# Fused attention and two feed-forward layers on one core: the order of VectorE's products with h and the lower parts of weights, and one W_out part on GpSimd

## The reference

```python
def _moe_ref(x, w_in, w_out):                 # layer 0
    h = x @ w_in
    g = h * np.clip(h + 3.0, 0.0, 6.0) / 6.0
    return (g @ w_out).astype(np.float32)

def _moe2_ref(x, w_in, w_out):                # layer 1
    h = x @ w_in
    sp = np.where(h > 20.0, h, np.log1p(np.exp(np.minimum(h, 20.0))))
    return ((h * np.tanh(sp)) @ w_out).astype(np.float32)

def reference(q, k, v, moe_w_in, moe_w_out, moe2_w_in, moe2_w_out):
    attn_out = _attn_ref(q, k, v)             # 4 x 8 heads, 576 x 64, block-causal softmax
    x = attn_out.transpose(0, 2, 1, 3).reshape(2304, 512)
    x = _moe_ref(x, moe_w_in, moe_w_out)      # 512 -> 2048 -> 512
    return _moe2_ref(x, moe2_w_in, moe2_w_out)
```

## Time and profile before

| | |
|---|---|
| median of 3 runs | 978.65 us (973.37 to 980.71) |
| the profiled execution | 975.95 us |
| its span | 974.0 us |
| TensorE busy | 952.0 us, 98% of the span |
| VectorE, ScalarE, GpSimd busy | 746.6, 643.6, 431.3 us |

### The profile page before, as it was taken

The page is one execution under the profiler, slowest core; times in us unless marked ns, Lnnn a source line. Parts: engine busy times, 40 slices in busy tenths (PEclk is TensorE's granted clock), DMA queues, the critical chain, the costliest instruction groups (busy, mean ns, idle before and its releaser), DMA issues.

```text
span 974.0 us, 17754 instructions
## 1 busy us (share of the span) xinstructions
PE 952.0 (98%) x6028; PEld 848.0 (87%) x6028; DVE 746.6 (77%) x1417; ACT 643.6 (66%) x1431; POOL 431.3 (44%) x410
## 2 busy tenths in 40 slices
PE   8999999999999999999899999999999999999998
PEld 7898888999887888888788988998998988988896
DVE  7898898774868686789788787777887777777654
ACT  7999999754544445454445557777777777776663
POOL 7899779665837596776867670000000000000000
PEclk9999999999999999999999999999999999999999
DMA  7988898657698978788786546555655654565255
GB/s 217 270 240 243 258 273 234 173 153 238 220 291 291 290 256 252 234 294 252 269 275 212 209 170 217 176 202 195 215 197 184 231 210 155 182 248 187 90 193 194
DMA packets 84601, 216.42 MB, mean 222 GB/s; under 512 B 10144, under 2 KB 16928, under 8 KB 84512
## 3 DMA queue, kind: packets, MB, share of 16 engines
q1 hardware_dynamic: 84368, 215.01, 67.6%
q10 hardware_dynamic: 144, 0.29, 0.1%
HBM read 162.07 MB, written 39.92 MB: 207 GB/s over the span
## 4 chain that ended last, share of the span: by engine, by line
PE 67%; DVE 7%; DMA 6%; SPq 4%; POOL 3%; issue 2%; ACT 1%; ACTq 0%; DVEq 0%; POOLq 0%
PE psum L1021 32%; PE psum L904 10%; PE psum L906 10%; PE psum L905 10%; DMA ext_d<-ext_made 3%; PE psum L849 2%; PE psum L828 2%; DVE ebuf L1624 1%; PE psum L808 1%; POOL osplit L1885 1%; SPq L646 1%; DVE glo L1630 1%; PE psum L809 1%; SPq L648 1%; DVE ext_made L1530 1%
## 5 line engine op out<-in xcount | busy, mean ns | idle before, releaser
L1021 PE MATMUL psum<-ghi,osplit 128*128 128x512 f32 (+1 forms) x640 | 216.7, 372 | 2.1 <-POOL osplit L1885 2.1
L904 PE MATMUL psum<-xhi,whi 128*128 128x256 f32 (+1 forms) x640 | 188.0, 294 | 5.1 <-ACT snap L1242 2.5
L906 PE MATMUL psum<-xhi,wlo 128*128 128x256 f32 (+1 forms) x640 | 187.2, 293 | 0.0
L905 PE MATMUL psum<-xlo,whi 128*128 128x256 f32 (+1 forms) x640 | 187.0, 292 | 0.0
L1021 PE MATMUL psum<-osplit,ghi 128*128 128x512 f32 x576 | 180.7, 395 | 1.3 <-DVE glo L1630 1.3
L1630 DVE SCALAR_TENSOR_TENSOR glo<-ebuf,ghi 128x512 fp32r<-128x512 f32 x144 | 126.5, 878 | 22.9 <-ACT ghi L1290 14.8
L904 PEld LDWEIGHTS psum<-xhi,whi 128*128 128x128 f32 x640 | 121.1, 189 | 19.0 <-ACT snap L1242 4.4
L1290 ACT ACTIVATE ghi<-ebuf 128x512 fp32r<-128x512 f32 x144 | 90.4, 628 | 66.9 <-DVE ebuf L1624 46.2
L1021 PEld LDWEIGHTS psum<-ghi,osplit 128*128 128x128 f32 x640 | 118.5, 190 | 18.4 <-issue 2.7
L1885 POOL TENSOR_TENSOR osplit<-oraw,osplit 128x512 fp32r<-128x512 f32 x80 | 117.2, 1468 | 38.1 <-ACT osplit L1209 34.0
L905 PEld LDWEIGHTS psum<-xlo,whi 128*128 128x128 f32 x640 | 121.2, 189 | 10.5
(11 more groups left out here) (120 smaller groups left out, 2147.4 us busy)
## 6 DMA issues: line engine op xcount, KB each, us to landing
ext<-ext_d SPq DMA_DIRECT2D x56, 768.0 KB, 4.4
osplit<-o_d SPq DMA_DIRECT2D x80, 512.0 KB, 5.3
oraw<-in_w_out SPq DMA_DIRECT2D x80, 256.0 KB, 5.8
wraw<-in_w_in SPq DMA_DIRECT2D x26, 512.0 KB, 6.0
ext_d<-ext_made SPq DMA_DIRECT2D x32, 384.0 KB, 6.2
attn_t<-ostage SPq DMA_DIRECT2D x32, 288.0 KB, 3.7
qkin<-in_qk SPq DMA_DIRECT2D x30, 288.0 KB, 3.7
kparts<-kparts SPq DMA_DIRECT2D x30, 288.0 KB, 4.2
```

The source lines that it names most:

```text
L904: pe.matmul(dst, hi, xh, start=(start and cc == 0), stop=False, skip_group_check=True)
L905: pe.matmul(dst, hi, xl, start=False, stop=False, skip_group_check=True)
L906: last = pe.matmul(dst, lo, xh, start=False, stop=(stop and cc == 1), skip_group_check=True)
L1021: last = pe.matmul(bank(Y_BANK + c, n), stat, mov, start=(first and m == 0), stop=(final and m == 2), skip_group_check=True)
```

## The change

VectorE: in `relu_period(s)` the two calls `extra_jobs(s - 1)` and `ahead_os(s - 1)` move behind both products with h and behind the low part of g of the first of the two tiles. GpSimd: in step 0 `mix_x(1, 1)`, the last sum of x for the wide block, moves behind the second `split_o`, that of tile 4. No instruction is added or taken away, and no wait is changed.

```diff
                 if first_of_block(s):
                     copy_y(BLOCK_OF[s] - 1, 3)
-                extra_jobs(s - 1)
-                ahead_os(s - 1)
                 relu6_times_h(s + 1, 0)
                 relu6_times_h(s + 1, 1)
                 split_g_lo(s + 1, 0)
+                extra_jobs(s - 1)
+                ahead_os(s - 1)
                 mixing_jobs(s)
...
                 if s == 0:
                     add_x(1, 3)
                     scale_x(1, 3)
-                    mix_x(1, 1)
                 next_x(s, 0)
                 for i in todo[1:2]:
                     split_o(i)
+                if s == 0:
+                    mix_x(1, 1)
                 next_x(s, 1)
```

## The result

The changed kernel takes 981.84 us in the median of 12 runs (978.29 to 983.53), the kernel before 975.73 us in 12 runs beside it (973.28 to 980.71). The ratio is 1.0066 with a 95% interval of 1.0050 to 1.0082: slower by 6.4 us, surely slower than before, and within the 1% that I took as no change. 982 was forecast. One further execution of the kernel before, in a later batch, took 1536 us at a granted clock of 0.557 and is in no ratio. The profiled spans are 974.0 us before and 979.5 us after, +5.5.

The account below looks back on a forecast made before the run. TensorE, busy in 98% of the span, bounds the kernel; its relevant waits are 10.3 us. Terms -3.6 + 2.8 + 2.7 - 1.8 + 3.7 + 0 = +3.8 us on the 978.65 median give 982; range 970 to 990.

Parts of the forecast that it names:

- Part 1: GpSimd in step 0: tile 4's low part before the mixing ends TensorE's 2.1 us wait and the low clock: -3.6 us.
- Part 2: VectorE's products earlier: waits for snap5, product and snap_3 end; -1.8 us before step 14, -4.9 in steps 20 to 26.
- Part 3: W_out loads in step 3: tile 16's load starts 6.9 us later, delaying copy_y and TensorE's bank: +2.8 us.
- Part 4: x loads in step 6: lower parts end 2.9 us later, so x reaches TensorE late; cover 0.2: +2.7 us.
- Part 5: x loads in step 14: released 4.15 us later, with nothing to cover it: +3.7 us, bounds 2.2 and 4.2.
- Part 6: x loads in step 22 come 3.3 us later, TensorE 1.9 later; with 2.0 won earlier kept, net about 0.
- Rival B: New long waits let TensorE's clock drop, 1.6 us each: up to 993 us; chance 0.23 beyond 1%, 0.2 inside.
- Rival A: TensorE's waits go and nothing takes their place: -10.4 to -11.4 us, 967 to 968; chance beyond 1% 0.12.
- Rival C: Only GpSimd's half shows; parts 3 to 6 come to what part 2 gives: -3.6, so 975 us; chance 0.2.
- the signs named in the forecast: snap5, snap_3 and step 0 waits gone; three x waits, some 10 us; x loads 3 and 4 us later; SyncE waits grow.
- theory 2: From the experiments, not the prediction: the order itself costs; the sums or the W_out tiles come late whenever x lands.

Follow-up runs that it names:

- run 1: Kernel before with only GpSimd's half: in step 0 the last x sum for the wide block moves behind tile 4's split; ratio 1.0016, 975.27 us.
- run 2: Kernel before with only VectorE's half: the lower parts of extra operands and W_out behind the products with h; ratio 1.0081, 982.24 us.
- run 9: Kernel before with ten one-element loads ahead of the x loads in steps 6, 14 and 22, no buffer added; ratio 1.0016, 976.48 us.
- run 10: Kernel before with ten one-element loads ahead of the W_in and W_out loads in steps 6, 14 and 22; ratio 1.0051, 980.34 us.
- Run 6: Changed kernel with VectorE's two lower parts between the first and second half's products with h; ratio 0.9969 to the kernel before, 974.03 us.
- run 11: Kernel before with VectorE's lower parts between the two halves' products with h, GpSimd's step 0 as before; ratio 0.9982, 973.71 us.
- run 12: Kernel before with one unused 16-element buffer ahead of the others, no instruction changed; ratio 1.0063, 981.32 us.
- run 8: Kernel before with an added 16-element buffer and five one-element loads ahead of the x loads in steps 6, 14 and 22; ratio 1.0051.

## Why the prediction was right, and where it was not

The time and its class came out: 982 forecast, 981.84 measured, and a shift of +6.4 us by the ratio where the sum said +3.8. Part of that is luck. First, the frame: the forecast was put on a median of 978.65 us from three executions, and the 12 beside the changed kernel have 975.73. The base was 2.9 us too high and the shift 2.6 us too small; on the later base the same sum gives 979.5. Second, several terms were off and made up for each other. What was right is the direction and the path: lower parts late on VectorE, SyncE's queue held up, x late, TensorE's first products of a block waiting for it.

- **Part 1, GpSimd in step 0: -3.6 forecast, -1.7 measured.** Mis-sized. Tile 4's low part no longer stood behind the mixing, but ScalarE's high part of tile 4 (L1209) ran only at 209.27, and TensorE waited 0.95 us for tile 4 and 0.37 for tile 5. "Nearly all goes, since 2.33 is more than 2.1" asked only for the old obstacle; I should have looked for the one behind it. And by runs 1 and 2 the gain is neither GpSimd's own nor one that lasts.
- **Part 2, the products earlier.** Of the -4.9 of steps 20 to 26, 2.0 were forecast to be won by step 22 and to stay: 1.4 was won from step 19 to 22, 1.95 to step 24. Of the -1.8 before step 14 the small one came (0.56 in step 12); the wait of 1.5 us for the first product (L1624) only shrank to 1.0.
- **Part 3, W_out loads in step 3: +2.8 forecast, +0.46 measured.** Mis-sized. Tile 16's load started at 241.17, not 242.8, and ScalarE could use it at 244.43, 3.3 us later. I had taken the page's median of 5.8 for a moment when the DMA engines were nearly idle (a share of 0.02 from 239.0 to 241.2); in the changed kernel that median itself is 4.8. The bound of 0.8 was not low enough.
- **Part 4, x loads in step 6: +2.7 forecast.** The low part of x came 2.1 us later where 2.9 was forecast, and TensorE lost 3.3 us in step 9 (from -1.22 to +2.04), since it arrived earlier. Another 2.04 us went in step 10 to the second wait and the slow clock, of which 0.56 came back in step 12. The size was about right, the cause half so: x was late because the W_in and W_out loads ahead of it were (runs 9 and 10), not because of its own issue. In the changed kernel both move together, which is why the sum came out.
- **Part 5, x loads in step 14: +3.7 forecast, +2.9 measured**, and of those a wait of 2.62 us and the slow clock behind it. x was 3.0 us later against the step where 4.15 was forecast.
- **Part 6, step 22: +1.9 forecast, +1.0 measured** (from step 24 to 28). x was 4.2 us later against the step where 3.3 was forecast, and the sum given for it, 4.4 less 1.3, is itself 3.1. The waits of 2.00 and 1.55 us stand where one of 4.8 was expected.
- **Rival B** was not a rival but a part of what happened. I gave the forecast no drops, and one or two of them a chance of 0.2. There were three stretches, one of them of double length, behind three of the four new long waits. Less the one of before that went, they made 3.7 of the 5.5 us. The Trainium skill's rule cited there ("TensorE: Matmul & The Clock Gate", section "What's actually happening"), that idleness brings the slow clock back, is borne out: the new stretches stand at waits of 3.02, 2.62 and 2.00 us, and none at that of 1.55. The wait of 2.32 us in the earlier trace rows had none, so the length of a single wait doesn't settle it.
- **Rival A** would have needed the lower parts to be free of followers. Run 6 is what is left of A: with the lower parts as early as before and one product in front, it is 0.3% faster.
- **Rival C**, that only GpSimd's half shows, is refuted by run 1, in which that half alone brought nothing.

What the signs named in the forecast showed: x loads 3.6 us later in step 6 and 3.0 in step 14 against the step (3 and 4 were named), SyncE's waits for VectorE grown, three waits for x (7.2 us where some 10 were named). The waits for snap_3 did not go; there is one of 2.00 us at 484.28, and it is the new order's own. VectorE's lower part had waited 1.55 us for its buffer and began at 477.23. Behind it stand three sums of W_in and then `add_c12` (L1612), which ran only at 482.79. ScalarE waited 1.67 us for it, up to 483.24, and copied snap_3 behind that. So the store's delay, which the old order put on snap5 (2.32 us), now falls on snap_3. At this place theory 2 is right: it costs without any late x, and the prediction's part 2 had taken it for won.

The summing itself was also at fault. A gain in TensorE's own time before step 9 doesn't simply add to a delay of x: in run 1 TensorE was 2.2 us ahead at step 6 and 0.4 behind at step 11. What an execution wins ahead of such a meeting point it may wait for there, and pay the clock for it.

Open: why the wait in step 0 is 2.1 us in some executions with the old order of GpSimd and 0.74 in another; why the slow clock follows one wait of 2 us and not another; and how much of the loss at steps 17 to 28 is late W loads, which run 10 did not make there.

## What to carry to other kernels

Before an instruction is moved back on an engine, list what its result frees: here a buffer, and with it the loads of W_in and W_out, on a queue in which later loads, in these traces, landed after them. Issuing the x loads 2.0 us later against the step behind the same W loads cost nothing that was measured (run 9); issuing the W loads late as well cost 4 us (run 10). If two things want to be first, put one piece of each: half the products, then the lower parts, then the rest was the only order that gained (runs 6 and 11, 0.3 and 0.2%). And count a wait on TensorE at its own length plus what the clock takes behind it.

## What the hardware showed that I had not expected

- One unused buffer of 64 bytes, which moves the later buffers, costs 0.6% (run 12): matmuls of 256 columns last 282 to 283 ns in place of 278 to 280, those of 512 columns 394 in place of 392. From step 28 on that came to 5.0 us, and in run 8 to 3.9. An experiment that adds a buffer needs a control with the buffer alone; run 8 would have been read as proof of the wrong theory.
- Single-element loads hold SyncE's queue for up to 0.34 us each (3.41 us for ten in step 6 of run 9, 3.25 in step 14), which makes them a means to delay what stands behind them.
- The same kernel runs with and without half-speed stretches. Of 76 executions of the kernel before, 34 have a mean granted clock of 1.000, 24 have 0.998 (one stretch, as in the profiled one) and 14 have 0.996 or less. The mean over many executions tells what one profile can't: by it the changed kernel loses some 3.6 us to the clock, and run 6 gains some 0.5 by it.
